# Mixture-of-experts kernel: gate logits carried through the attention, expert rows gathered by a table

## The chip, the cores and the metric

One core of one Trainium2 chip. The metric is the device time of one run in microseconds, the median of several runs. The kernel before has 408.28 us (three runs, 408.23 to 409.46).

## What is computed

Three stages follow each other. A linear attention with a decaying state gives 1536 tokens of 384 features (2 batches, 8 heads, 768 positions, 48 features a head). A mixture of experts sends each token to the expert with its largest logit, at most 384 tokens an expert, in order of the tokens. A dense layer with h - tanh(h) follows.

```python
for t in range(S):                               # attention
    cur = einsum('bhd,bhe->bhde', u[None] * kt, vt)
    y[:, :, t] = einsum('bhd,bhde->bhe', rt, state + cur)
    state = w[None, :, :, None] * state + einsum('bhd,bhe->bhde', kt, vt)
...
logits = x @ w_gate                              # experts: N=1536, D=384, E=8, F=1024
expert_idx = argmax(logits, axis=1)
gate_w = softmax(logits)[arange(N), expert_idx]
for i in range(N):
    e = expert_idx[i]
    if counts[e] < capacity:
        disp[e, counts[e]] = x[i]; pos[i] = counts[e]; counts[e] += 1; keep[i] = True
h = maximum(einsum('ecd,edf->ecf', disp, w1), 0)
y = einsum('ecf,efd->ecd', h, w2)
out[i] = gate_w[i] * y[expert_idx[i], pos[i]]    # where kept
...
h = x @ w_in; out = (h - tanh(h)) @ w_out        # dense, d_ff = 2048
```

## The kernel before

**Attention.** Twelve steps n, each a tile of 128 tokens of all eight heads; steps 0 to 5 are the first batch, 6 to 11 the second. TensorE runs in each step, in the order of its program: score products into pA (L1140, L1144), the state update pT (L1165, not in steps 5 and 11), queries times state (L1174) and later scores times values (L1189) into pY, the "own" products with u for the next step (`own_products`, L1105), the transposes of the x of the step before (`x_transposed`, L1084), the transposed own rows (`own_transposed`, L1116), and the logits of the step before (`logits`, L1094). VectorE writes the weighted queries (`queries`, L792), the masked scores (L880), the weighted keys (`keys`, L784), the state (L890, L892) and x (`output`, L859). GpSimd multiplies r and k (`products`, L481), makes the keys for the state (`end_keys`, L489) and v times the own term (vdiag, L507). ScalarE scales queries and state, and copies out of PSUM. SP issues the loads (`feature_part`, `token_part`, `value_part`).

**Routing.** Tiles are routed in groups, 4, 4, 2, 2. `route1` finds a tile's expert from the logits, `route2` the gate and the place in the expert; ROUTE1, ROUTE2, SCALED and SENT say in which step that, the scaling of x by the gate (`scale_x`, ScalarE) and the sending happen. Groups 2 and 3 come at the end of the attention. x goes to the tensor x_by_slot in HBM, where a row's address is its expert and place: ScalarE fills it with zeros by nine transfers of 576 KB (L650), GpSimd scatters the rows of each tile by an indirect DMA (`scatter`, L472). SP loads an expert's 384 rows by one plain transfer (`expert_rows`).

**Between attention and experts.** Rows of tiles 0 to 7 for expert 0 are loaded (`loaded`, L1211). Those of tiles 8 to 11 are taken straight from SBUF: VectorE writes one-hot matrices (`spots_of`, L837) and TensorE multiplies x by them (`direct`, L1205). ScalarE and VectorE split the result in a high and a low part (`split_x`, L939).

**Experts.** For each expert TensorE does `first` (three products of high and low parts for each block), transposes the next expert's rows (`transposed_rows`, L1254), and does `second`. Weights go HBM to four raw buffers, ScalarE makes the high part (L580), VectorE the low part of W1 (L849), GpSimd that of W2 (`low`, L460). In experts 0 and 1 GpSimd also scatters six tiles' token numbers each by rank (`token_ranks`, L521). Each engine runs its own instructions in the order of its program; all order between engines is by semaphores written by hand.

The steps of the prediction touch these names and lines, the queue of GpSimd above all.

Of the kernel before, what the change touches and what calls it, by code (L numbers as in the profile page):

```python
# [21 lines left out]
ALU = mybir.AluOpType  # L22
# [7 lines left out]
P = 128  # L30
# [10 lines left out]
REF = 32  # L41
KD = D // P
# [5 lines left out]
XS = 10  # L48
# [5 lines left out]
ZP = 9  # L54
# [11 lines left out]
def build(nc, by_feature_d, by_token_d, w_d, u_d, wg_d, w1_d, w2_d, out_d):  # L66
    xs_d = nc.dram_tensor("x_by_slot", (E * CAP + N, D), F32, kind="Internal").ap()
# [3 lines left out]
    with ctx:  # L71
# [26 lines left out]
        limit = sb("slot_limit", [P, GS], F32)  # L98
# [4 lines left out]
        sloti = sb("sloti", [P, NG, GS], I32)  # L103
# [14 lines left out]
        large_i = sb("large_i", [P, 1], I32)  # L118

# [3 lines left out]
        kv = sb("kv", [P, 3, 2, D], F32, att)  # L123
# [7 lines left out]
        vdiag = sb("vdiag", [P, D], F32, att)  # L131
        diag = sb("diag", [P, 2, H], F32, att)
        own_rows_sb = sb("own_by_head", [P, P], F32, att)
        st = sb("st", [P, 2, NP, DH], F32, att)
        stw = sb("stw", [P, NP, DH], F32, att)
        x = sb("x", [P, XS, D], F32, att)
        xT = sb("xT", [P, KD, P], F32, att)
        early = sb("early", [P, 1], F32, att)
        wcol = sb("wcol", [P, NP], F32, att)
        ucol = sb("ucol", [P, NP, 2], F32, att)  # L140
        wgate = sb("wgate", [P, KD, E], F32, att)
        pw = sb("powers", [P, NP, 2 * REF + P], F32, att)
        kendt = sb("kendt", [P, NP, 2, HALF], F32, att)
# [3 lines left out]
        zero_row = x[:, XS - 1, :]  # L147
# [38 lines left out]
        u_in = sem("u_in")  # L186
        wgate_in = sem("wgate_in")
        feature_in = [sem(f"feature_in{i}") for i in range(3)]
        token_in = [sem(f"token_in{i}") for i in range(3)]
# [8 lines left out]
        xs_zero = sem("xs_zero")  # L198
# [20 lines left out]
        lg_full = sem("lg_full")  # L219
        lg_done = sem("lg_done")  # L220
# [3 lines left out]
        xt_full = sem("xt_full")  # L224
        xt_done = sem("xt_done")
# [10 lines left out]
        scat = [sem(f"scattered{i}") for i in range(STEPS)]  # L236
# [93 lines left out]

        def place(n):
# [6 lines left out]
        def expert_rows(e):  # L338
            return xs_d[bass.ds(e * CAP, CAP), :].rearrange("(b p) d -> p b d", p=P)
# [12 lines left out]
        def _(sp):  # L352

            def feature_part(n):
                if n < 3:
                    sp.dma_start(rkT[:, n], by_feature_d[n]).then_inc(feature_in[n], 16)
                else:
                    sp.wait_ge(e_ready, n - 2)
                    sp.wait_ge(kw_ready, n - 2)
                    sp.wait_ge(rk_ready, n - 2)  # L360
                    for par in range(2):
                        rows = slice(par * HALF, par * HALF + DH)
                        sp.dma_start(rkT[rows, n % 3], by_feature_d[n, rows]).then_inc(feature_in[n % 3], 16)

            def token_part(n):
# [4 lines left out]
                sp.dma_start(kv[:, n % 3, 0], by_token_d[n, :, 0]).then_inc(token_in[n % 3], 16)  # L370

            def value_part(n):
# [4 lines left out]
                sp.dma_start(kv[:, s, 1], by_token_d[n, :, 1]).then_inc(value_in[s], 16)  # L377
# [11 lines left out]
            sp.dma_start(ucol[:, :, :], u_d).then_inc(u_in, 16)  # L389
# [4 lines left out]
            sp.dma_start(wgate[:, :, :], wg_d.rearrange("(c p) e -> p c e", p=P)).then_inc(wgate_in, 16)  # L394
# [12 lines left out]
            unit(2, 0, 0)  # L407
            unit(2, 0, 1)
# [980 lines left out]
```

## Time and profile before

| what | value |
|---|---|
| median of three runs | 408.28 us |
| the profiled execution, its own time | 410.51 us |
| its span, first to last instruction | 408.8 us |
| TensorE busy | 384.9 us, 94% |
| VectorE busy | 214.2 us, 52% |
| ScalarE busy | 180.9 us, 44% |
| GpSimd busy | 155.7 us, 38% |
| granted TensorE clock, mean | 0.980 |
| moved by DMA | 56.85 MB, 139 GB/s |

PE is TensorE's product, PEld its weight load, DVE VectorE, ACT ScalarE, POOL GpSimd, SP SyncE. The granted clock is a share of 2.4 GHz; 0.50 is 1.2 GHz. The shares are means over the whole span; the stages differ much.

### The profile page before, as it was taken

To read this page: it belongs to the slowest core of one execution; us is meant where nothing else is said; L and a number is where in the kernel's file an instruction comes from. 1 tells how busy PE (TensorE), PEld (TensorE's weight loads), DVE (VectorE), ACT (ScalarE), POOL (GpSimd) and SP (SyncE) were. 2 spreads that over 40 slices of the span, in tenths; PEclk is the share of its full clock that TensorE was granted. 3 is DMA by queue.
4 is the path that set the end of the run, shared out by engine and by line. 5 is a ranking of instruction groups with operands and counts; after the bars stand their busy time and mean duration, and the time that the engine had idled before them with its cause. 6 is when DMAs were issued, how large, how long until landed. Compare 5 with 4: busy or idle time off the path is not lost.

```text
span 408.8 us, 10468 instructions
## 1 busy us (share of the span) xinstructions
PE 384.9 (94%) x3738; PEld 373.1 (91%) x3739; DVE 214.2 (52%) x453; ACT 180.9 (44%) x486; POOL 155.7 (38%) x132
## 2 busy tenths in 40 slices
PE   7999898698999999999999899999999999999991
PEld 7777687598999999999999899999999999999991
DVE  7667978574555655555465356615252434343340
ACT  5553456434564665756656454533022313231220
POOL 3966665435877742715517051541002000110002
PEclk9999999689999999999999999999999999999997
DMA  7989986444849478576684527000000000010001
GB/s 246 271 251 269 249 211 220 141 149 154 264 162 285 150 249 261 189 253 192 224 284 158 182 79 226 6 21 38 0 0 19 38 0 0 0 58 0 0 0 65
DMA packets 41541, 56.85 MB, mean 139 GB/s; under 512 B 3584, under 2 KB 39104, under 8 KB 41504
## 3 DMA queue, kind: packets, MB, share of 16 engines
q1 hardware_dynamic: 35936, 46.23, 36.9%
q10 hardware_dynamic: 3600, 5.31, 4.1%
q0 software_dynamic: 1968, 4.83, 3.1%
q8 instruction: 22, 0.36, 0.4%
q14 instruction: 15, 0.12, 0.1%
HBM read 46.23 MB, written 10.13 MB: 138 GB/s over the span
## 4 chain that ended last, share of the span: by engine, by line
PE 58%; issue 18%; POOL 13%; DVE 4%; DMA 2%; ACT 2%; another core or an unknown queue 1%; POOLq 0%; DVEq 0%; SPq 0%; ACTq 0%
POOL w_lo L460 11%; PE ring L1065 9%; PE ring L1067 9%; PE ring L1066 9%; PE pO L1317 8%; PE pO L1316 8%; PE pY L1189 2%; POOL token_of_rank L521 2%; PE ring L1205 2%; PE pA L1140 2%; PE pD L1094 1%; DVE At L880 1%; PE pY L1174 1%; PE pX L1084 1%
## 5 line engine op out<-in xcount | busy, mean ns | idle before, releaser
L460 POOL TENSOR_TENSOR w_lo<-raw_weights,w_hi 128x768 fp32r<-128x768 f32 x40 | 73.5, 1846 | 84.6 <-ACT w_hi L580 84.3
L1007 DVE SCALAR_TENSOR_TENSOR minus_tanh<-square,ring 128x384 f32<-128x384 f32 x64 | 35.5, 554 | 93.5 <-ACT square L730 79.1
L580 ACT ACTIVATE w_hi<-raw_weights 128x768 fp32r<-128x768 f32 x80 | 67.1, 848 | 28.5 <-DMA raw_weights<-w 28.4
L730 ACT ACTIVATE square<-ring 128x384 f32<-128x384 f32 x64 | 31.4, 491 | 94.7 <-DVE h_hi L1017 53.8
L1065 PE MATMUL ring<-yT_hi,w_hi 128*128 x192 | 65.0, 339 | 1.7 <-DVEq L1002 1.7
L1316 PE MATMUL pO<-w_hi,h_hi 128*128 128x384 f32 x192 | 64.9, 338 | 0.0
L1317 PE MATMUL pO<-w_lo,h_hi 128*128 128x384 f32 x192 | 64.8, 338 | 0.0
L1066 PE MATMUL ring<-yT_lo,w_hi 128*128 x192 | 64.8, 338 | 0.0
L1067 PE MATMUL ring<-yT_hi,w_lo 128*128 x192 | 64.8, 338 | 0.0
L1065 PE MATMUL ring<-xT_hi,w_hi 128*128 128x224 f32 x192 | 52.9, 275 | 1.6 <-issue 1.1
L849 DVE TENSOR_TENSOR w_lo<-raw_weights,w_hi 128x768 fp32r<-128x768 f32 x40 | 42.4, 1073 | 22.3 <-ACT w_hi L580 18.7
L550 POOL DMA_INDIRECT out<-out_rows,tok x12 | 11.7, 976 | 111.1 <-ACT out_rows L725 107.2
L1065 PE MATMUL pO<-h_hi,w_hi 128*128 128x224 f32 x192 | 53.2, 277 | 0.0
L1067 PE MATMUL ring<-xT_hi,w_lo 128*128 128x224 f32 x192 | 52.6, 274 | 0.6 <-issue 0.6
L1066 PE MATMUL ring<-xT_lo,w_hi 128*128 128x224 f32 x192 | 52.6, 274 | 0.0
L1067 PE MATMUL pO<-h_hi,w_lo 128*128 128x224 f32 x192 | 52.6, 274 | 0.0
L1066 PE MATMUL pO<-h_lo,w_hi 128*128 128x224 f32 x192 | 52.6, 274 | 0.0
L967 DVE SCALAR_TENSOR_TENSOR h_lo<-ring,h_hi 128x224 fp32r<-128x224 f32 x64 | 24.3, 390 | 32.9 <-ACT h_hi L697 30.9
L1065 PEld LDWEIGHTS ring<-xT_hi,w_hi 128*128 128x128 f32 x192 | 36.8, 192 | 2.8 <-issue 2.0
L1065 PEld LDWEIGHTS ring<-yT_hi,w_hi 128*128 128x128 f32 x192 | 36.0, 188 | 1.9 <-issue 1.9
L1065 PEld LDWEIGHTS pO<-h_hi,w_hi 128*128 128x128 f32 x192 | 36.8, 192 | 0.1
L1067 PEld LDWEIGHTS pO<-h_hi,w_lo 128*128 128x128 f32 x192 | 36.9, 192 | 0.0
(158 smaller groups left out, 744.1 us busy)
## 6 DMA issues: line engine op xcount, KB each, us to landing
raw_weights<-w SPq DMA_DIRECT2D x80, 384.0 KB
x_by_slot<-x ACTq DMA_DIRECT2D x9, 576.0 KB, 4.4
x_expert<-x_by_slot SPq DMA_DIRECT2D x8, 576.0 KB
kv<-kv_by_token SPq DMA_DIRECT2D x22, 192.0 KB, 4.2
rkT<-rk_by_feature SPq DMA_DIRECT2D x18, 192.0 KB, 5.1
rkT<-rk_by_feature SPq DMA_DIRECT2D x3, 512.0 KB, 4.5
x_expert<-x_by_slot SPq DMA_DIRECT2D x1, 384.0 KB
x_by_slot<-x,sloti POOLq DMA_INDIRECT x12, 4.1
```

The lines of the kernel that those rows point to most:

```text
L460: pool.tensor_tensor(lo, unit_raw(2, k), hi.bitcast(F32), ALU.subtract).then_inc(w2_ready, 1)
L550: pool.indirect_dma_start(out=out_d, out_offset=bass.IndirectOffsetOnAxis(ap=tok3[:, i:i + 1], axis=0), in_=ost[:, i, :], in_offset=None). ...
L580: act.activation(hi, unit_raw(what, k), ACT.Copy).then_inc(w1_hi if what == 1 else w2_hi, 1)
L730: act.activation(sq[:, i % 2, :], ring[i % 4][:, 0:CAP], ACT.Square, scale=THIRD ** 0.5, accum_out=sqsum[:, bass.ds(t * (2 * FC) + i, 1)]) ...
L849: dve.tensor_tensor(lo, unit_raw(1, k), hi.bitcast(F32), ALU.subtract).then_inc(w1_ready, 1)
L967: dve.scalar_tensor_tensor(out=hl[:, f, 0:cols], in0=ring[f % 4][:, 0:cols], scalar=0.0, in1=hh[:, f, 0:cols].bitcast(F32), op0=ALU.max, o ...
L1007: dve.scalar_tensor_tensor(out=nt[:, i % 2, :], in0=sq[:, i % 2, :], scalar=1.0, in1=ring[i % 4][:, 0:CAP], op0=ALU.subtract, op1=ALU.mult ...
L1065: pe.matmul(out, hi, m_hi, start=first, stop=False)
L1066: pe.matmul(out, hi, m_lo, start=False, stop=False)
L1067: return pe.matmul(out, lo, m_hi, start=False, stop=last)
L1316: pe.matmul(pO[k][:, 0:D], g, W2h[:, s, f, :], start=starts, stop=False)
L1317: last = pe.matmul(pO[k][:, 0:D], g, W2l[:, s, f, :], start=False, stop=(ends and not general))
```

## The change

The logits are no longer computed from the finished x. The gate's weights multiply v ahead of the attention (together with the own products, with v by feature as one more input), and each head's eight logits stand behind its 48 values, in a row of 64 with room (`gated_values`). The attention carries them as it does the values, so that x comes out as 56 columns a head, and VectorE sums the eight logits over the heads (`owners_of`). The transposes of x, the logit products and their copies go.

x is stored by token (x_d, SP, twelve plain transfers) and not by slot; the zero fill goes but for one row. A table of the row of each slot is made by products of one-hot matrices (`tabled`), the matrices by GpSimd for tiles 0 to 3, one tile in each of steps 8 to 11 (`spread`, SPREAD), and by VectorE for the others. GpSimd gathers the rows of every expert by three indirect DMAs (`gather`, `expert_rows`). These stand in GpSimd's order behind the low parts and the rank scatters of an expert.

The routing groups are 4, 4, 4. The work of a group is cut in four pieces (`owners_of`, `counts_of`, `route2`, `places_of`) in different steps. The low parts of W1 of expert 0 move behind the attention.

```diff
-GROUPS = [(0, 4), (4, 4), (8, 2), (10, 2)]
+GROUPS = [(0, 4), (4, 4), (8, 4)]
-ROUTE1 = {5: 0, 9: 1}
+OWNERS = {4: 0, 8: 1}
+COUNTS = {5: 0, 9: 1}
 ROUTE2 = {6: 0, 10: 1}
-SCALED = {8: [0, 1], 9: [2, 3], 11: [4, 5, 6, 7]}
-SENT = {9: [0, 1], 10: [2, 3], 11: [4, 5, 6, 7]}
+PLACES = {7: 0}
+SPREAD = {8: 0, 9: 1, 10: 2, 11: 3}
+SCALED = {7: [0], 8: [1], 9: [2], 10: [3], 11: [4, 5, 6, 7]}
...
@@ sync
-            for n in range(DIRECT):
-                sp.wait_ge(scat[n], 16)
-            sp.dma_start(xe[:, 0:2, :], expert_rows(0)[:, 0:2, :]).then_inc(xe_in, 16)
...
+            for n in range(STEPS):
+                sp.wait_ge(xg_ready, n + 1)
+                sp.dma_start(x_d[1 + n * P:1 + (n + 1) * P, :], row(n)).then_inc(stored[n], 16)
+            for k in range(4):
+                unit(2, 0, k)
             with sp.Fori(0, E - 1) as e:
                 for k in range(4):
                     unit(1, e + 1, k)
-                sp.wait_ge(ring_full, e * RING + (RING + KD))
-                sp.dma_start(xe[:, :, :], expert_rows(e + 2)).then_inc(xe_in, 16)
...
@@ gpsimd
+            def spread(n):
+
+                pool.wait_ge(places_ready, 1)
+                pool.tensor_scalar(qhot[:, n, :], counts[:, :], reached[:, n:n + 1], tokno[:, n:n + 1], ALU.is_equal, ALU.mult)
+                pool.tensor_scalar(phot[:, n, :], lanes[:, :], lane_no[:, n:n + 1], None, ALU.is_equal
+                                   ).then_inc(pool_hot_ready, 1)
...
+            def gather(source, rows, k, landed):
+
+                pool.sem_inc(passed, 1)
+                pool.indirect_dma_start(
+                    out=xe[:, k, :], out_offset=None, in_=source,
+                    in_offset=bass.IndirectOffsetOnAxis(ap=rows[:, k:k + 1], axis=0)).then_inc(landed, 16)
+
+            def expert_rows(e):
+
+                pool.tensor_copy(row3[:, :], row_i[:, e, :]).then_inc(row3_made, 1)
+                pool.wait_ge(row3_made, e)
+                for k in range(BLOCKS):
+                    gather(x_d, row3, k, xe_in)
...
                 for n in range(e * C, (e + 1) * C):
                     token_ranks(n)
-            with pool.Fori(1, E // 2 + 1) as j:
+                pool.wait_ge(ring_full, e * RING + (RING + KD))
+                expert_rows(e + 2)
...
@@ vector
+                gated = x[:, first % XS:first % XS + m, :].rearrange("p i (h e) -> p i e h", h=H)
+                link(dve.tensor_reduce(logit[:, 0:m], gated[:, :, DH:DV, :], AX.X, ALU.add))
...
+                if n == STEPS - 1:
+                    places_of(1, rlink)
...
+            spread(1)
             output(STEPS - 1)
+            owners_of(2, rlink)
+            counts_of(2, rlink)
             route2(2, rlink)
-            spots_of(8)
...
+            for n in range(DIRECT, STEPS):
+                spots_of(n)
+            places_of(2, rlink)
+            spread(2)
+            low(0, 0, 0)
...
@@ tensor, own_products
+                    pe.matmul(pX[32 * p:32 * p + 2 * E + 2, D:D + P], own_gate[:, 0, p, :], rkf[:, p, :],
+                              start=True, stop=False, skip_group_check=True)
+                pe.wait_ge(vfeature_in[n % 3], loaded_features(n))
+                for p in range(NP):
+                    last = pe.matmul(pX[32 * p:32 * p + 2 * E + 2, D:D + P], own_gate[:, 1, p, :], vT[:, n % 3, p, :],
+                                     start=False, stop=True, skip_group_check=True)
...
+            pe.wait_ge(pool_hot_ready, DIRECT // 2)
+            pe.wait_ge(hot_ready, 1)
+            tabled(range(DIRECT))
+            pe.wait_ge(diag_ready, STEPS)
+            keep_warm(8, ones[:, :], pX[:, 0:P])
+            pe.wait_ge(x_ready, STEPS)
+            positions(2)
```

## Rows read from the trace of the kernel before

**Rows 1.** Windows by stage: length, busy us of each engine (instructions), clock, DMA share, GB/s
```profile
14.70:70.40 55.70, 51.22 (x1265) 43.07 (x1264) 44.80 (x87) 29.04 (x117) 36.81 (x32) 1.00 0.84 239
...
92.90:228.90 136.00, 134.92 (x1200) 134.20 (x1200) 74.30 (x147) 82.43 (x175) 73.08 (x45) 1.00 0.69 219
```

**Rows 2.** Chain of waits, one attention step: start us, length us, what
```profile
25.97 0.21 PE pA L1140
...
26.99 0.60 PE pT L1165 x16
27.59 0.61 PE pY L1174 x32
28.20 0.33 PE pX L1105 x8
28.54 0.48 PE pX L1084 x3
29.01 1.07 PE pY L1189 x32
...
30.34 0.57 PE pD L1094 x6
```

**Rows 3.** Timeline and groups of instructions, GpSimd in the attention
```profile
28.71 1.37 POOL L481 TENSOR_TENSOR rkf<-rkT 128x512 f32<-128x512 f32 x1 [1.47 <-PE pX L1105]
...
35.42 1.01 POOL L489 TENSOR_TENSOR kend<-kv,kendt 128x384 f32<-128x384 f32 x1
...
L489 POOL TENSOR_TENSOR kend<-kv,kendt 128x384 f32<-128x384 f32 x8 | 9.8, 1226 | 0.0
```

**Rows 4.** Timeline, VectorE, routing in the attention
```profile
39.49 1.07 DVE L800 TENSOR_TENSOR ldiff<-logit,lmax 128x32 f32<-128x32 f32 x1
...
61.27 0.18 DVE L799 TENSOR_REDUCE lmax<-logit 128x4 f32<-128x32 f32 x1
61.48 0.19 DVE L800 TENSOR_TENSOR ldiff<-logit,lmax 128x32 f32<-128x32 f32 x1
```

**Rows 5.** Timeline, TensorE, from the last attention step to the experts
```profile
72.92 1.14 PE L1189 MATMUL pY<-kv,At 128*64 128x48 f32 x32 [0.52 <-DVE At L880]
...
80.93 4.08 PE L1205 MATMUL ring<-kw,x 128*128 128x224 f32 x10
...
86.69 1.48 PE L1211 MATMUL ring<-ident,x_expert 128*128 128x128 f32 x12
88.00 2.46 PE L1205 MATMUL ring<-At,x 128*128 128x224 f32 x12
...
92.94 0.36 PE L1065 MATMUL ring<-xT_hi,w_hi 128*128 128x224 f32 x1 [1.14 <-issue]
```

**Rows 6.** Timeline, VectorE, the same stretch
```profile
77.48 0.55 DVE L859 TENSOR_TENSOR x<-vdiag,pY 128x384 f32<-128x384 f32 x1 [2.03 <-remote]
...
79.22 0.75 DVE L837 TENSOR_SCALAR kw<-At,token_slot 128x384 f32<-128x384 f32 x2
...
90.51 0.99 DVE L939 TENSOR_TENSOR xT_lo<-ring,xT_hi 128x224 fp32r<-128x224 f32 x3
```

**Rows 7.** Timeline, GpSimd, in experts 0 and 1
```profile
105.16 1.52 POOL L521 DMA_INDIRECT token_of_rank<-tokrow,rank_i  x1
...
112.39 0.96 POOL L521 DMA_INDIRECT token_of_rank<-tokrow,rank_i  x1 [0.30 <-issue]
115.67 7.26 POOL L460 TENSOR_TENSOR w_lo<-raw_weights,w_hi 128x768 fp32r<-128x768 f32 x4 [2.32 <-ACT w_hi L580]
...
130.86 0.96 POOL L521 DMA_INDIRECT token_of_rank<-tokrow,rank_i  x1 [0.30 <-issue]
```

**Rows 8.** Timeline of TensorE, and GpSimd's scatters of x by tile
```profile
136.43 0.82 PE L1254 MATMUL ring<-ident,x_expert 128*128 128x128 f32 x6
...
DMA to landing us min/median/max: 3.3/4.1/7.3
```

**Rows 9.** Windows of one microsecond, columns as in the first group
```profile
75.00:76.00 1.00, 0.80 (x6) 0.70 (x6) 0.45 (x1) 0.00 (x0) 0.93 (x1) 0.69 0.52 197
```

More of the change, by code:

```diff
@@ L41 @@
 REF = 32
+DV = DH + E
+WIDE = HALF
+BLOCKS = CAP // P
+Q = E * BLOCKS
 KD = D // P
@@ L513, in _ @@
                               allow_small_or_imprecise_dtypes=True).then_inc(slots_ready, 1)
-                for i in SENT.get(n, []):
-                    scatter(i)
-            for n in range(DIRECT, STEPS):
-                scatter(n)
+                if n in SPREAD:
+                    spread(SPREAD[n])
+            def gather(source, rows, k, landed):
[8 more added lines that the diff above has]
+                    gather(x_d, row3, k, xe_in)
+            pool.wait_ge(table_done, 1)
+            link(pool.tensor_copy(early_i[:, :], table[:, 0, 0:BLOCKS]))
+            pool.wait_ge(zero_in, 16)
+            for n in range(DIRECT):
+                pool.wait_ge(stored[n], 16)
+            gather(x_d[0:1 + DIRECT * P, :], early_i, 0, xe_in)
+            gather(x_d[0:1 + DIRECT * P, :], early_i, 1, xe_in)
+            gather(x_d[0:1 + DIRECT * P, :], early_i, 2, xe_rest_in)
+            pool.wait_ge(table_done, 2)
+            link(pool.tensor_tensor(table[:, 2, :], table[:, 0, :], table[:, 1, :], ALU.add))
+            link(pool.tensor_copy(row_i[:, 0:E, :].rearrange("p e k -> p (e k)"), table[:, 2, :]))
+            for n in range(DIRECT, STEPS):
+                pool.wait_ge(stored[n], 16)
+            pool.wait_ge(xe_rest_in, 16)
+            pool.wait_ge(ring_full, KD)
+            pool.wait_ge(meta_ready, 1)
+            with pool.If(tokens_of(pool, 0) > NARROW):
+                pool.wait_ge(wide_full, KD)
+            expert_rows(1)
             def token_ranks(n):
@@ L535, in _ @@
                         low(j * 2 + s, k, s)
+                    pool.wait_ge(ring_full, (j * 2 + s) * RING + (RING + KD))
+                    pool.tensor_copy(row3[:, :], row_i[:, bass.ds(j * 2 + (s + 2), 1), :].rearrange("p a k -> p (a k)")
+                                     ).then_inc(row3_made, 1)
+                    pool.wait_ge(row3_made, j * 2 + (s + 2))
+                    for k in range(BLOCKS):
+                        gather(x_d, row3, k, xe_in)
+            for e in range(E - 2, E + 2):
+                for k in range(4):
+                    low(e, k, e % 2)
+                if e == E - 2:
+                    pool.wait_ge(ring_full, e * RING + (RING + KD))
+                    expert_rows(E)
             pool.wait_ge(rank_sc, STEPS * 16)
@@ L622, in decayed_state, with table_copy @@
                     last.then_inc(stw_ready, 1)
+            def table_copy(g):
+                act.wait_ge(table_full, g + 1)
+                act.copy(table[:, g, :], pD[:, 0:Q]).then_inc(table_done, 1)
             def decayed_queries(n):
@@ L809, in route1, with counts_of @@
                                        bc(owners.unsqueeze(2), [P, m, E]), ALU.is_equal))
+            def counts_of(g, link):
+                first, m = GROUPS[g]
+                owners = allf[:, 0, first:first + m]
                 for i in range(m):
@@ L1125, in positions, with tabled @@
                           start=False, stop=True).then_inc(pos_full, 1)
+            def tabled(tiles):
+                for n in tiles:
+                    last = pe.matmul(pD[:, 0:Q], phot[:, n % DIRECT, :], qhot[:, n % DIRECT, :], start=(n == tiles[0]),
+                                     stop=(n == tiles[-1]))
+                last.then_inc(table_full, 1)
             for n in range(STEPS):
```

348 lines of the change are left out of this document (158 added, 190 removed).

## The prediction

> **What bounds the kernel now.** I read the windows view first, cut where the work changes. From 14.7 to 70.4 us run the attention steps 1 to 10 (step n begins with its score products): TensorE is busy 51.2 of 55.7 us, VectorE 44.8, GpSimd 36.8, and the DMA engines 84%. From 92.9 to 228.9 us the eight experts run with TensorE busy 134.9 of 136.0 us; behind them lies the dense part, which the change leaves alone. So whatever is won ahead of the experts shortens the run, unless an expert then has to wait [rows 1]. The chain of waits gives one undisturbed attention step: scores from 25.97, state update 0.60, state times queries 0.61, own products 0.33, transposes of x 0.48, values 1.07, own transpose, logits 0.57 ending at 30.91, so 4.94 us of TensorE without a hole [rows 2]. Ten steps of it are 49.4 us of the 55.7; the other 6.3 us are late VectorE work around the routing and short holes. Then comes the piece between attention and experts: the last value products start at 72.92 and end at 74.06, the first expert product starts at 92.94. I call these points Y (end of the last value products) and F. F minus Y is 18.9 us [rows 5].
>
> **Profiled run and median.** Its span is 408.8 us and its own time 410.51 us, the median of the runs 408.28 us. The sum below is made in that span as a difference, and goes onto the median.
>
> **The attention step.** Removed from TensorE: the transposes of x (0.48) and the logits (0.57). Added: the own products now also take four products with v, as many as there were, so 0.33 more [rows 2]. The operands of state and value products widen from 48 to 64 columns. The records do not scale with columns there: the 32 value products take 33 ns each start to start, two at a time on different columns of the array, and the full-width score products run beside the 64-column ones in the same time. I take 0 for the widening; the other bound is a third of 0.60 + 0.61 + 1.07, that is 0.76 us a step. TensorE is then at 4.94 - 0.48 - 0.57 + 0.33 = 4.22 us. But something else is late next. GpSimd starts the r times k product 0.18 us after the own products end (28.53 to 28.71), its end-keys follow 1.2 us later and take 1.01, or 1.23 on average, and the state update waits for them [rows 2, 3]. That loop is 0.18 + 1.2 + 1.01 + 0.1 + 0.60 + 0.61 + 0.66 = 4.36 us, 4.6 with the mean duration. I take 4.5 us a step, 45 for ten; bounds 4.36 and 4.98 (TensorE with the whole widening).
>
> GpSimd also gets the one-hot rows of a tile in each of steps 8 to 11, two single-input operations of 24 and 128 columns. Nothing in the trace has that form on GpSimd; the nearest are its 1.37 us for 512 columns with two inputs and 1.01 for 384 [rows 3], so 0.3 to 0.7 us together. They stand ahead of the next r times k product, but GpSimd has a hole there, and I count them at nothing; without the hole they would cost 4 times 0.7 at most.
>
> VectorE: x is 448 instead of 384 wide, under 0.1 us. Routing comes in pieces after the state copy. A small operation takes 0.18 us and the next starts 0.21 later, but one that meets GpSimd took 1.07 [rows 4]. Owners of four tiles is now seven operations with the added sum over heads, about 2.0 us; counts, gates and places about 1.2 each. The hole after the state copy in a 4.5 us step is about 1.1 us (VectorE busy 44.8 of 55.7 us now). So each owners piece puts 0.9 us on the path, about 1.7 with a collision like the 1.07, and the others 0.2 to 0.4: 4.5 us for all. Short holes of the kind seen now I keep at 3 us. The front grows 0.5 us through the longer own products and five more constants. Step 11 needs 0.9 us more, since the places of the second group stand ahead of its score copy. Sum: 45 + 4.5 + 3 + 0.5 + 0.9 = 53.9 against 55.7: **-1.8 us** to Y (from -5 to +3 with the bounds). The zero fill leaves 9 transfers of 576 KB off the DMA engines, 5.3 MB, against 3.2 MB of v twice more; both ride on queues that no step waits for now, so 0. SP issues two more transfers a step and the stores of x, all inside its idle time, since it waits for the steps.
>
> The Trainium skill, "SBUF — State Buffer", section "Who interferes with whom", says that a VectorE operation with two SBUF inputs and a GpSimd one that reads SBUF block each other. The 1.07 us fits. By that rule alone each of the spread routing pieces could wait for one GpSimd operation, which makes the attention about 5 us longer than my sum.
>
> **Between Y and F.** Now VectorE writes x only at 77.48 after 2.03 us of waiting for something unnamed [rows 6], and GpSimd was then sending rows out; those scatters go. The new order from Y: x done Y+0.75; owners, then counts Y+3.3; position products, Y+4.1; positions summed Y+4.6; four spot matrices at 0.375 each (0.75 for two) [rows 6]: Y+6.1. TensorE starts the gathering products at Y+5.2. It has 24 records of 224 columns (12 products), and 12 took 2.46 us at full clock [rows 5], so Y+9.9; then the products with the loaded rows, 1.48 for 12 [rows 5], Y+11.2. The two gathers of loaded rows start on GpSimd at about Y+3 and land by Y+8.5, in time. VectorE goes on from Y+6.1: places 1.2, one-hots 1.2, w low part 0.9, counts 1.7, tail values 0.6, w low part 0.9, three splits of 0.33 [rows 6], so Y+13.8. TensorE needs the table products, 4 warm products and 1.1 us for the branch: F = Y+14.4. Against 18.9 this is **-4.5 us**. Two low parts of W1 that now ride inside the attention are counted here, and the two behind F end before the fifth block of the first expert asks for them.
>
> **Behind F.** Expert rows now come by three GpSimd gathers each, not by one transfer from SP. They stand in GpSimd's queue behind the low parts of W2 and, in experts 0 and 1, behind six scatters of token ranks each; queued behind them are the next low parts, which TensorE's second products need. Now: six ranks from 105.16 to 113.35, low parts 115.67 to 122.93, six ranks up to 131.82 [rows 7]. New, counted from F (92.94 now): ranks end F+20.4; three gathers at 1.3 us apart to F+24.6, in a hole of which 2.3 us were free; low parts 7.3, F+31.9; six ranks 8.8, F+40.7; a copy and a wait 0.4; the last gather starts F+43.7. A scatter of the same 192 KB lands 3.3 to 7.3 us after its start, median 4.1 [rows 8], so the rows are there at F+47.8. TensorE wants them for the transposes of expert 3 at 136.43, F+43.5 [rows 8]. Nothing behind can give this back, as TensorE has 1.1 idle us in 136 [rows 1]. So **+4.3 us** (3.5 to 7.5), about 1 of it already at expert 2. From expert 4 on GpSimd has no ranks, and its 7.3 + 4.3 us fit into the 16.7 of an expert.
>
> The Trainium skill, "DMA: Bandwidth & Descriptors", section "Anatomy of one DMA — SWDGE (gpsimd) path", gives 2.0 us and the bytes over 436 GB/s, 2.45 us for such a gather. Its landing would then be F+46.2 and the stall 2.7 us, and the result 404.8 us. The 4.1 of the trace decides here.
>
> **Sum.** -1.8 - 4.5 + 4.3 = -2.0; 408.3 - 2.0 = **406.3 us**.
>
> **Rivals.**
> - *The clock falls again behind Y.* Now it falls within 75 to 76 us (mean 0.69 in that microsecond, so from 2.4 to 1.2 GHz inside it), after some 3.5 us in which TensorE had only 1.1 us of full products and small ones, and records of the gathering products then take 0.41 us [rows 5, 9]. The new stretch has 1.9 idle us ahead of the value products (late score copy), 1.1 us of them, then 24-column table products, and only then eight warm ones. For the fall: so little work. Against: the stretch is some 2 us shorter. Price: positions about 2 us later behind slow warm products, and gathering records at 0.41 us each (10 took 4.08) instead of 0.205 (12 took 2.46) [rows 5] for some of them, 1 to 3 us: +3.5 us, so 409.8 us. It decides once the clock is at 1.2 GHz before Y+3.
> - *Slower: VectorE and GpSimd become the bound of the attention.* If a collision meets most routing pieces and the widening costs its 0.76, Y is not 1.8 us earlier but 3 later: -2.0 + 4.8 gives 411.1 us. It decides when the step passes 5.1 us. For: the 1.07 for 0.19 us. Against: the widened records are not bound by columns.
> - *The gathers are covered.* If they land in 2.5 us and the ranks in their shortest spacing, the stall is 2 us, and with a step at 4.36 the result is 402.6 us. For: fewer bytes on the queues. Against: nothing in rows 8 is under 3.3.
>
> **Chances.** My forecast's case 0.37, the clock 0.25, the slow attention 0.18, the covered gathers 0.20. About 0.3% (1.2 us) is what a measurement of this kernel can tell from no change. The forecast's own case scatters by 2 us, so 0.24 of it lies below 407.1 and the rest near none; the covered gathers are faster in full; of the clock 0.06 is within and 0.19 slower; the slow attention is slower but for 0.03. Faster 0.44, same 0.22, slower 0.34. Range: 402.0 to 412.5, which leaves out the outer parts of the last two cases.
>
> **What would show it.** Steps 1 to 4 at 4.4 to 4.6 us with the state update waiting for GpSimd's end-keys; VectorE full in steps 4 and 8; clock at 1.0 through Y+3 to Y+11; F some 14 us behind Y; TensorE idle before the transposes of experts 2 (about 1 us) and 3 (about 3), released by an indirect transfer, and nowhere else among the experts. Wrong if the wide products lengthen the step, if the ranks leave room for the gathers, or if the clock falls.

## The result and the profile after

The changed kernel takes 416.73 us (median of four, 414.48 to 419.38), the kernel before 408.25 us beside it (four, 405.47 to 409.46). The ratio is 1.022, with a 95% interval of 1.013 to 1.031: slower by 8.5 us, where 2 us faster had been forecast, and outside the forecast range.

The profiled execution took 418.18 us, the one of the kernel before 410.51 us; each column of the table below is one execution. Three points carry the comparison, all read from TensorE's timeline: Y, the end of the last value products; F, the first expert product; and D, the first product of the dense part. D stands at 230.6 us before and at 238.51 after.

| us | before | after | difference | forecast |
|---|---|---|---|---|
| Y | 74.06 | 76.16 | +2.1 | -1.8 |
| F minus Y | 18.88 | 15.74 | -3.1 | -4.5 |
| D minus F | 137.7 | 146.6 | +8.9 | +4.3 |
| behind D | 178.2 | 177.9 | -0.3 | 0 |
| sum (spans 408.8 and 416.4) | | | +7.6 | -2.0 |

First the stages of the kernel after (windows: stretch, length, busy us of TensorE, its weight loads, VectorE, ScalarE, GpSimd with instructions, clock, DMA share, GB/s), to be laid beside [rows 1]:

```profile
14.70:70.40 55.70, 46.77 (x1246) 37.98 (x1244) 49.17 (x85) 25.64 (x107) 38.48 (x35) 0.97 0.73 196
...
92.90:228.90 136.00, 129.53 (x1126) 128.69 (x1124) 72.64 (x145) 79.57 (x166) 101.78 (x75) 0.97 0.68 209
```

In the attention TensorE works 4.5 us less in the same window and VectorE 4.4 us more; among the experts TensorE, busy 134.9 of 136.0 us before, is now idle or slow, and GpSimd's busy time rises from 73.1 to 101.8 us. The largest waits of TensorE that are new or have grown are these (total us, times, longest):

```profile
PE ring L1317 <- DMA x_expert<-x_by_token,row: 5.5, 2, 3.7
PE pY L1256 <- DVE At L953: 4.3, 6, 2.0
PE pY L1245 <- issue: 3.3, 3, 1.5
```

**Among the experts.** The rows arrive by a transfer, so the transfer is named. The chain of waits that ended last (each piece followed back to what released it) names the real cause. From just ahead of F it leaves TensorE and stays in GpSimd's queue for 46 us (start, length, what; the longest pieces):

```profile
92.24 0.90 POOL row L543
...
98.07 7.23 POOL w_lo L484 x4
105.47 1.54 POOL token_of_rank L570
...
119.22 7.11 POOL w_lo L484 x4
126.50 1.53 POOL token_of_rank L570
...
138.60 3.85 DMA x_expert<-x_by_token,row
142.57 1.43 PE ring L1317 x6
```

Low parts, six rank scatters, three gathers; again low parts, scatters, gathers; then one gather's landing, and TensorE. A full turn of this queue takes 21.0 us (105.47 to 126.50), while TensorE turns an expert round in 16.7 once nothing disturbs it (transposes of two later experts at 160.99 and 177.72). So the queue loses 4.3 us in each turn with rank scatters. What reaches TensorE is read from its transposes. Those of expert 2 come at F+30.4 instead of F+26.3 (119.20 us before), 4.1 us late, and those of expert 3 at F+50.7 instead of F+43.5, 7.2 us late (timeline; the wait is in brackets):

```profile
122.26 1.54 PE L1317 MATMUL ring<-ident,x_expert 128*128 128x128 f32 x6 [3.72 <-DMA x_expert<-x_by_token,row]
...
142.57 1.43 PE L1317 MATMUL ring<-ident,x_expert 128*128 128x128 f32 x6 [1.75 <-DMA x_expert<-x_by_token,row]
```

**The clock behind a wait.** The granted clock, a share of 2.4 GHz, falls when work comes back. Windows of one microsecond behind the second wait:

```profile
142.00:143.00 1.00, 0.43 (x3) 0.44 (x4) 0.00 (x0) 0.00 (x0) 1.00 (x1) 0.86 0.12 28
143.00:144.00 1.00, 1.00 (x7) 1.00 (x5) 0.40 (x2) 0.69 (x2) 1.00 (x2) 0.50 0.99 340
...
146.00:147.00 1.00, 1.00 (x10) 1.00 (x10) 1.00 (x1) 0.14 (x1) 1.00 (x2) 0.93 0.67 207
```

The engine sat idle from 140.8 to 142.6 us and then ran at 1.2 GHz for some 3.2 us. Summing what the windows fall short of 1.00 gives 1.7 us, and the next transposes come 18.4 us later (142.57 to 160.99) instead of 16.7: the same 1.7. With the 7.2 us above this gives the 8.9 of the table. The fall behind the first wait is as deep, but adds nothing, since GpSimd's queue sets the time of the second wait anyway.

**In the attention.** The start of VectorE's masked-score copy marks the steps. From step 4 to step 10 it takes 33.6 us before (32.01 to 65.63) and 34.9 after. The five profiles that have this attention (this one and those of experiments 1, 3, 4 and 5 below) lie between 34.8 and 35.5 us, the two that have the attention before at 33.2 and 33.6, so this difference is clear of the scatter. Y is not as firm: 77.35 us in the second profile of the attention before, where the clock was at 0.50 from 26 to 32 us. VectorE's timeline after:

```profile
32.17 1.31 DVE L953 COPY_PREDICATED At<-before,pA 128x1024 f32<-128x1024 uint32 x1
...
40.35 2.60 DVE L867 TENSOR_TENSOR upto<-upto,onehot 128x8 f32<-128x8 f32 x4
...
59.23 0.80 DVE L854 SCALAR_TENSOR_TENSOR score<-ldiff,prio 128x32 f32<-128x32 f32 x1 [0.16 <-DVE ldiff L851]
...
63.79 1.89 DVE L867 TENSOR_TENSOR upto<-upto,onehot 128x8 f32<-128x8 f32 x4
...
67.08 1.29 DVE L953 COPY_PREDICATED At<-before,pA 128x1024 f32<-128x1024 uint32 x1
```

Four additions of eight columns take 2.60 and 1.89 us here. The first such chain took 0.77 us in the kernel before (at 42.00), and it takes 0.77 behind the attention of this one (78.77), where GpSimd is nearly idle. The chain of waits has the four additions singly, and GpSimd's timeline what it ran beside them:

```profile
40.43 1.17 DVE upto L867
...
41.62 0.94 DVE upto L867
...
42.58 0.18 DVE upto L867
```

```profile
39.90 1.66 POOL L491 TENSOR_TENSOR rkf<-rkT 128x512 f32<-128x512 f32 x1 [0.48 <-PE pX L1166]
41.52 1.00 POOL L499 TENSOR_TENSOR kend<-k_tok,kendt 128x384 f32<-128x384 f32 x1
```

The first addition ends at 41.60, GpSimd's product at 41.56; the second ends at 42.56, GpSimd's end-keys at 42.52. With GpSimd idle behind them the others take 0.18 us. From 45 to 60 us VectorE has no room left:

```profile
45.00:60.00 15.00, 12.14 (x331) 9.90 (x331) 14.50 (x27) 8.04 (x35) 11.68 (x11) 1.00 0.71 171
```

It is busy 14.50 of 15 us, where it was 12.69 before, and TensorE is busy only 12.14. In the first steps the changed kernel loses what it had gained: TensorE has a hole of 1.53 us at 17.07 ("issue", no releaser in the trace), the clock is at 0.50 from 20 to 23 us, and at step 4 the two kernels are level (32.01 and 32.17). Where the hole is missing, in experiment 9, step 4 begins at 30.82. A hole of 1.47 us at 66.95 is followed by no fall of the clock.

**Between Y and F.** TensorE's timeline, to be laid beside [rows 5]:

```profile
75.01 1.15 PE L1256 MATMUL pY<-v_and_gate,At 128*64 128x64 f32 x32 [1.96 <-DVE At L953]
...
78.19 3.50 PE L1146 MATMUL pX<-ones 128*128 128x128 f32 x16
...
83.02 2.54 PE L1266 MATMUL ring<-kw,x 128*128 128x224 f32 x12 [0.75 <-DVE kw L915]
85.39 2.43 PE L1266 MATMUL ring<-At,x 128*128 128x224 f32 x12
87.66 1.47 PE L1272 MATMUL ring<-ident,x_expert 128*128 128x128 f32 x12
...
91.90 0.37 PE L1138 MATMUL ring<-xT_hi,w_hi 128*128 128x224 f32 x1 [0.51 <-DVE xT_lo L1010]
```

The gathering products run at full speed, 12 in 2.54 and 2.43 us, where ten took 4.08. The warm products ahead of them ran at 1.2 GHz, 3.50 us for sixteen records. That fall cost a microsecond or so, as the runs below show by difference.

The 3.1 us won here should not be put down to the change alone. In the profile of before the clock is at 0.50 from 76 to 85 us, in that of after only from 78 to 81; summed as above, the fall takes 5.1 us of full clock there and 1.7 here, a difference as large as the gain. The stretch is also uneven from run to run in the kernel before: 20.7 us in experiment 2, and 14.4 in experiment 10, where Y was late and the fall behind it was short. What the change gives between Y and F at an equal clock is not shown.

### The profile page after: what moved, and what is told of

Read it like the earlier page. It is cut to its first block, busy times and chain, and to the rows that moved or that the text cites. A ratio compares the mean times of both kernels' runs of the same rounds, so it can differ in the third digit from the quotient of the medians.

```text
span 416.4 us, 10595 instructions
## 1 busy us (share of the span) xinstructions
PE 383.1 (92%) x3774; PEld 371.1 (89%) x3775; DVE 225.0 (54%) x454; ACT 178.0 (43%) x474; POOL 186.5 (45%) x171
## 4 chain that ended last, share of the span: by engine, by line
PE 70%; POOL 10%; DVE 10%; issue 5%; DMA 1%; ACT 1%; POOLq 0%; DVEq 0%; ACTq 0%
PE ring L1138 11%; PE ring L1139 11%; PE ring L1140 11%; PE pO L1379 8%; PE pO L1380 8%; PE pO L1139 4%; PE pO L1138 4%; PE pO L1140 4%; POOL token_of_rank L570 4%; POOL w_lo L484 3%; DVE At L953 2%; PE pY L1256 2%; POOL x_expert L537 1%; DVE rw L841 1%; DVE kw L833 1%
## 5 line engine op out<-in xcount | busy, mean ns | idle before, releaser
L1080 DVE SCALAR_TENSOR_TENSOR minus_tanh<-square,ring 128x384 f32<-128x384 f32 x64 | 35.5, 554 | 92.5 <-ACT square L779 92.5
L922 DVE TENSOR_TENSOR w_lo<-raw_weights,w_hi 128x768 fp32r<-128x768 f32 x40 | 43.4, 1099 | 20.8 <-ACT w_hi L643 20.2
L1138 PE MATMUL pO<-h_hi,w_hi 128*128 128x224 f32 x192 | 54.3, 283 | 0.0
L1139 PE MATMUL pO<-h_lo,w_hi 128*128 128x224 f32 x192 | 53.5, 279 | 0.0
L1138 PEld LDWEIGHTS pO<-h_hi,w_hi 128*128 128x128 f32 x192 | 38.0, 198 | 0.2 <-issue 0.2
L1138 PEld LDWEIGHTS ring<-yT_hi,w_hi 128*128 128x128 f32 x192 | 36.1, 188 | 2.1 <-issue 1.9
L1139 PEld LDWEIGHTS pO<-h_lo,w_hi 128*128 128x128 f32 x192 | 37.9, 198 | 0.0
```

The costliest lines, as they stand in the source:

```text
L922: dve.tensor_tensor(lo, unit_raw(1, k), hi.bitcast(F32), ALU.subtract).then_inc(w1_ready, 1)
L1080: dve.scalar_tensor_tensor(out=nt[:, i % 2, :], in0=sq[:, i % 2, :], scalar=1.0, in1=ring[i % 4][:, 0:CAP], op0=ALU.subtract, op1=ALU.mult ...
L1138: pe.matmul(out, hi, m_hi, start=first, stop=False)
L1139: pe.matmul(out, hi, m_lo, start=False, stop=False)
```

## The experiments

The theory by then: the time among the experts is lost because the gathers stand behind the rank scatters on GpSimd, and the time in the attention because VectorE is full, partly with operations that GpSimd makes slow. Ratios are to the kernel before on the same chip and carry the 95% interval. The scatter of single runs of either kernel is 1.5 to 2%, so the positions in the traces weigh more here than the medians.

**1. The rank scatters out of experts 0 and 1, in the changed kernel.**

```diff
-                if e == 0:
-                    pool.wait_ge(rank_ready, 1)
-                for n in range(e * C, (e + 1) * C):
-                    token_ranks(n)
                 pool.wait_ge(ring_full, e * RING + (RING + KD))
                 expert_rows(e + 2)
...
                 if e == E - 2:
                     pool.wait_ge(ring_full, e * RING + (RING + KD))
                     expert_rows(E)
+                    pool.wait_ge(rank_ready, 1)
+                for n in {E - 2: range(0, 2), E - 1: range(2, 8), E: range(8, STEPS)}.get(e, []):
+                    token_ranks(n)
```

> The changed kernel; only the twelve scatters of token ranks leave experts 0 and 1 on GpSimd's queue and run behind the low parts of experts 6, 7 and 8 (two, six, four). Theory (the expert rows are late because their gathers stand behind the rank scatters): no wait for a gather before the transposes, no fall of TensorE's clock among the experts, first expert product to first dense product 138 to 139 us instead of 146.6, the whole some 8 us under the changed kernel, 408 to 409.5 us, so level with the kernel before. Rival (three gathers an expert on GpSimd are too slow in themselves, or the stage is long for contention): the stretch stays over 142 us and the whole over 413.

Measured: 414.57 us against 413.33, ratio 1.0047 (1.0001 to 1.0092). From F (92.55) to D (231.36) 138.8 us instead of 146.6, and TensorE's waits hold none for the gathers. The 7.8 us are the scatters' place in the queue. By the ratios of this run and of the changed kernel (1.0047 and 1.022) the whole gains 1.7%, some 7 us.

**2. The same move in the kernel before.**

> The kernel before with the same move of the rank scatters. Its GpSimd has holes around them and nothing of TensorE waits for it, so the theory expects at most 1 us (its first two expert periods are 17.41 and 17.23 us against 16.72 later): 407 to 408.5 us. If rank scatters slow TensorE in themselves, through the DMA engines or ports, the two periods fall to 16.7 and the whole by more than 1 us.

Measured: 418.75 us, ratio 1.0118 (1.0044 to 1.0192), F to D 140.8 us. TensorE's period from expert 2 to expert 3 is 17.17 us, 17.23 before, so the scatters do not slow TensorE in themselves, and the move gains next to nothing where nobody waits for GpSimd, as expected. The loss was not expected. Part of it lies ahead of F (98.04 instead of 92.94), where the edit changes nothing and the clock was at 0.50 for longer (26 to 32 and 81 to 93 us). The other 3.1 us lie at the entry of the dense part:

```profile
234.31 0.35 ACT L709 CAST yT_hi<-pO 128x224 f32 x1 [1.54 <-PE pO L1070]
235.77 0.35 ACT L709 CAST yT_hi<-pO 128x224 f32 x1 [1.11 <-remote]
237.22 0.35 ACT L709 CAST yT_hi<-pO 128x224 f32 x1 [1.10 <-remote]
```

ScalarE's three copies of the last expert's result stand 1.45 us apart, while GpSimd issues six rank scatters from 228.14 to 236 us. Before they ran in 1.03 us together (from 228.37). What holds them ("remote", not an engine of the trace) is not settled; that it is the scatters is argued from the same time and from experiment 3.

**3. All twelve scatters in the dense part.** As 1, but with

```diff
-                for n in {E - 2: range(0, 2), E - 1: range(2, 8), E: range(8, STEPS)}.get(e, []):
+                for n in {E: range(0, 8), E + 1: range(8, STEPS)}.get(e, []):
```

> The changed kernel; all twelve rank scatters in the dense part, eight behind the low parts of its first half, four behind those of its second. With the scatters in experts 6 to 8 the three copies of expert 7's result came 0.3 to 0.7 us apart instead of at once and the stretch to the first dense product was 138.9. If indirect transfers being issued slow those copies, the stretch is now 137.5 to 138.2 us; if not, 138.9 again.

Measured: 411.83 against 410.99, ratio 1.0059 (1.0010 to 1.0107), F to D 137.1 us (92.49 to 229.62). The three copies run in 1.03 us again. So the whole difference among the experts is explained, and taken back, by the place of the scatters.

**4. As 3, with sixteen more warm records of TensorE ahead of the last value products.**

```diff
+                if n == STEPS - 1:
+                    keep_warm(8, ones[:, :], pD[:, P:2 * P])
                 pe.wait_ge(a_done, n + 1)
```

> The same, and TensorE runs eight warm products while it waits for the late score copy of step 11. Now its clock falls to 1.2 GHz from 77.9 to 81.1 us and the position products are ready only at 82.1, 2 us after VectorE asks for them. If idle time ahead of the last value products lets the clock fall, it stays at 1.0 here, the gathering products start about 1.7 us earlier and the first expert product comes 14 to 14.5 us behind the end of the last value products instead of 15.7. The rival, that the small table products behind it are what lets it fall, leaves 15.7. Whole: 1 to 3 us under the kernel before on the same chip if the first holds, level with it otherwise.

Measured: 410.81 us, ratio 0.9998 (0.9947 to 1.0048), level with the kernel before and not 1 to 3 us under it. The clock stays at 1.0 behind Y:

```profile
80.00:81.00 1.00, 1.00 (x11) 1.00 (x11) 0.93 (x3) 0.00 (x0) 0.00 (x0) 1.00 0.00 0
```

F minus Y is 14.7 us (79.61 to 94.27); Y itself is late, in part because the clock was at 0.79 from 60 to 76 us already, ahead of the edit, and in part because the new records (76.48 to 78.5) still ran when the score copy was done at 77.3. The experiment doesn't show that the warm records hold the clock: it also held behind Y in 3 and 5, without them. F minus Y is 14.6 and 14.3 there; in the changed kernel and in 1, where it fell, 15.7 and 15.9. The forecast 14.4 was right for the full clock, and the fall costs 1.3 us, not the 3.5 of the rival.

**5. The gathers ahead of the scatters.** Is it the order in the queue, or its length?

```diff
-                for n in range(e * C, (e + 1) * C):
-                    token_ranks(n)
                 pool.wait_ge(ring_full, e * RING + (RING + KD))
                 expert_rows(e + 2)
+                for n in range(e * C, (e + 1) * C):
+                    token_ranks(n)
```

> The changed kernel; in experts 0 and 1 the three gathers stand ahead of the six rank scatters instead of behind them. If the order alone is the trouble, the waits for gathers go and first expert product to first dense product falls to about 139 us, as with the scatters moved away. My theory says that the amount on GpSimd's queue is: four low parts 7.3, six scatters 9.2 and three gathers 4.2 us are 20.7 us in an expert of 16.7, so now the low parts of W2 of experts 1 and 2 come late, TensorE waits for them some 2 to 5 us in all, and the stretch is 141 to 144 us, against 146.6 with the gathers last.

Measured: 417.49 us, ratio 1.0178 (1.0080 to 1.0277), F to D 145.4 us. The gathers are in time, and no wait names them. But now the low parts behind the scatters are late, and TensorE waits for them:

```profile
140.82 0.37 PE L1138 MATMUL pO<-h_hi,w_hi 128*128 128x224 f32 x1 [2.96 <-POOL w_lo L484]
```

The clock is at 0.50 behind this wait too, from 142 to 144. Only 1.2 of the 8.9 us come back, less than the forecast of 141 to 144 us said. It is the length of the queue, not its order: 21.0 us of work against 16.7.

**6. GpSimd's one-hot rows behind the attention.** A rival of "VectorE is full" was that this new work of GpSimd slows the attention.

```diff
-                if n in SPREAD:
-                    spread(SPREAD[n])
...
+            for i in range(DIRECT // 2):
+                spread(i)
             pool.wait_ge(table_done, 1)
```

> The changed kernel; GpSimd makes the one-hot rows of tiles 0 to 3 behind the attention, not one tile in each of steps 8 to 11. It takes 1.5 us a step (0.46 and 1.0) ahead of the r times k product. If that delays the attention, the last value products end 2 us or more earlier than 76.2; if VectorE sets the pace there, as I think, they end under 1 us earlier, and the four tiles in a row (some 4.5 us) come out behind as a later table and no gain of the whole.

Measured: 420.57 us, ratio 1.0253 (1.0144 to 1.0362). Steps 4 to 10 take 34.8 us (34.9), and Y is at 76.6. F minus Y grows to 19.7 us, since the table products wait for the rows (2.0 us) and the clock is then at 0.50 from 78 to 84. One of the slow chains turns fast, as GpSimd is quiet there:

```profile
60.09 0.19 DVE L854 SCALAR_TENSOR_TENSOR score<-ldiff,prio 128x32 f32<-128x32 f32 x1 [0.16 <-DVE ldiff L851]
...
65.11 0.75 DVE L867 TENSOR_TENSOR upto<-upto,onehot 128x8 f32<-128x8 f32 x4
```

Yet the steps are no shorter: VectorE is busy 14.59 us from 45 to 60 as before. The collisions move to the key products (1.75 us at 63.11 for an operation that else takes 0.67), since the r times k product and the end-keys of GpSimd stay. The one-hot rows themselves are not the cause.

**7 and 8. One more operation of VectorE a step, in both kernels** (an unused reduction, in steps 1 to 10).

```diff
+                if 1 <= n <= 10:
+                    dve.tensor_reduce(spare[:, n, :], pw[:, :, 0:P], AX.X, ALU.max)
```

> The changed kernel with one more single-input VectorE operation (a maximum over 512 columns, about 0.6 us) behind the state copy in each of steps 1 to 10; its result is used by nothing. Theory (VectorE is the bound of the attention since the change): the end of the last value products moves from 76.2 us by 4 to 6 us, as only the first steps have a hole. Rival (the loop over GpSimd's end-keys or TensorE is the bound, VectorE has a hole of 1.1 us a step): it moves by under 2 us.

> The same additional VectorE operation in the kernel before. Theory (TensorE is the bound there, VectorE has a hole except in the routing steps): the end of the last value products moves from 74.1 us by under 2.5 us. If it moves by 4 to 6 as well, VectorE was the bound before already and the change's loss in the attention has to be read as VectorE work added to a full engine.

Measured: 421.75 us, ratio 1.0201 (1.0082 to 1.0321), and 418.63 us, ratio 1.0126 (0.9990 to 1.0262). Steps 4 to 10 grow by 1.2 us in both, from 34.9 to 36.1 and from 33.6 to 34.9, for six operations of 0.68, 4.1 us. Y moves by 3.0 and 1.9 us. By Y this did not tell the theories apart: it was to cost 4 to 6 us in the one and under 2.5 in the other. VectorE's busy time in steps 4 to 10 says more. In the changed kernel it grows by only 1.1 us (33.45 to 34.56), as other operations met GpSimd less (the two chains take 2.02 and 1.50 us, not 2.60 and 1.89), and the steps grow by as much. In the kernel before it grows by 2.8 us (28.23 to 31.01) and the steps by less than half of that. What VectorE is not busy in these six steps is 1.3 to 1.5 us in all nine profiles of changed kernels in this document, whatever was added or taken away, and 3.9 to 5.4 us in the four of the kernel before and its variants. In the changed kernel the steps follow VectorE.

**9 to 11. Less work for VectorE, with the same result.** The four chained additions of a group's running counts become a copy and a reduction over overlapping windows of five rows.

```diff
-        onehot = sb("onehot", [P, GS, E], F32)
+        window = sb("window", [P, 4 + GS, E], F32)
+        onehot = window[:, 4:4 + GS, :]
...
+            dve.memset(window[:, 0:3, :], 0.0)
...
-                for i in range(m):
-                    link(dve.tensor_tensor(upto[:, first + i + 1, :], upto[:, first + i, :], onehot[:, i, :], ALU.add))
+                link(dve.tensor_copy(window[:, 3, :], upto[:, first, :]))
+                five = window[:, 0:m, :]
+                five = bass.AP(five.tensor, five.offset, [five.ap[0], [E, m], [1, E], [E, 5]])
+                link(dve.tensor_reduce(upto[:, first + 1:first + m + 1, :], five, AX.X, ALU.add))
```

> The changed kernel, with the four chained additions of each group's running counts (in the trace of the changed kernel 2.60 us at 40.35 us and 1.89 us at 63.79 us, 0.77 us behind the attention) replaced by one copy and one reduction over overlapping windows, both with a single tensor input; an estimate for the two together is 0.6 us (a copy of 8 columns 0.17, a reduction of 96 to 128 columns 0.26 to 0.4). Nothing is left out. Theory VectorE sets the attention's pace in the changed kernel: about 3.3 us of its work go, and the last value products end 2.5 to 3.5 us earlier (73 to 74 instead of 76.2 us), the whole 2 to 3.5 us shorter. Rival, VectorE is only busy beside what sets the pace (TensorE with its clock, or the chain through ScalarE): the last value products end within 0.8 us of 76.2. First expert product to first dense product stays at 146 to 147 us by both.

> The kernel before with the same replacement (there the chains took 0.77 us at 42.00 and 1.76 us at 62.50 us, and 0.37 us each behind). Theory VectorE sets the pace only in the changed kernel: VectorE idles 1 to 3 us in every 15 us of this attention, and the end of the last value products moves by less than 0.8 us from 74.1; the whole within 1 us of the kernel before. Rival, VectorE sets the pace in both: 1.3 to 2 us earlier.

> The changed kernel with all twelve rank scatters in the dense part and the window reduction for the running counts. If both causes are the ones named and they add up: first expert product to first dense product 137 to 138 us, last value products at 73 to 75 us, and the whole 2 to 3 us below the version with only the scatters moved (which stood at 1.0059 of the kernel before), so about 0.995 to 1.000 of the kernel before. If VectorE is not what sets the attention's pace: 1.004 to 1.007 again.

Measured in the changed kernel: 414.95 us, ratio 1.0112 (1.0030 to 1.0193). Its VectorE:

```profile
30.82 1.32 DVE L957 COPY_PREDICATED At<-before,pA 128x1024 f32<-128x1024 uint32 x1
...
38.97 1.25 DVE L868 COPY window<-upto 128x8 f32<-128x8 f32 x1
40.26 0.45 DVE L871 TENSOR_REDUCE upto<-window 128x32 f32<-128x160 f32 x1
...
61.68 0.25 DVE L868 COPY window<-upto 128x8 f32<-128x8 f32 x1
61.96 0.44 DVE L871 TENSOR_REDUCE upto<-window 128x32 f32<-128x160 f32 x1
...
64.22 1.29 DVE L957 COPY_PREDICATED At<-before,pA 128x1024 f32<-128x1024 uint32 x1
```

The work went from 2.60 + 1.89 to 1.70 + 0.69 us, 2.1 less and not the 3.3 expected, because a copy with one input can meet GpSimd too (1.25 us). Steps 4 to 10 take 33.4 us, 1.5 less, which is what the kernel before needs (33.6). Y is at 74.09; 1.3 us of that gain are only the missing fall of the clock in the first steps (step 4 at 30.82). In the kernel before, the same edit leaves steps 4 to 10 at 33.9 us (33.21 to 67.10). So with less work for VectorE the steps get shorter in the changed kernel and not in the kernel before: VectorE is the bound after the change and was not before. The run of the kernel before is a weaker control than was meant, since one operation that met GpSimd (1.83 us at 62.77 for 0.19) took the saving away, and VectorE was busy 29.06 us in steps 4 to 10, not less than 28.23. From F to D this run took 143.4 us, less than the 146 to 147 expected. Its first low parts start at F+4.9 instead of F+6.2, several indirect transfers are issued in 1.0 instead of 1.6 us, and the clock holds behind the second wait (the waits are 2.38 and 1.39 us).

The kernel before with windows: 408.3 us, ratio 0.9928 (0.9882 to 0.9974), the fastest of all. Its Y was to stay within 0.8 us of 74.1 and is at 78.55, with the clock at 0.50 from 68.5 to 78; F is at 92.93, as before (92.94). The 3 us by which its profiled span is shorter lie behind D (175.7 us against 178.2), where the edit changes nothing: the products of the dense part take 334 ns each there and 338 in the profile before. So the gain of 0.7% is not shown to come from the windows. The changed kernel with windows and with all scatters in the dense part: 409.28 us, ratio 0.9959 (0.9924 to 0.9994), F to D 137.4 us, as expected, and steps 4 to 10 in 32.7. Y was expected at 73 to 75 us and is at 77.1, because TensorE stands still for 3.8 us ("issue") from 63.4 on in a step that VectorE, ScalarE and GpSimd wait through as well. F minus Y is 17.6 us there: TensorE waited 2.06 us for a gather of the first expert's rows, issued at 82.21 and there at 89.2, and the clock fell behind that wait (0.50 from 91 to 97). Both repairs together put the changed kernel 0.4% ahead of the kernel before. It remains behind or level with the kernel before once that has windows too.

## Why the prediction was wrong, step by step

**The gathers (+4.3 forecast, +8.9 measured).** The mechanism was right, the size was not. The prediction had the last of the second three gathers start at F+43.7; it starts at F+46.7 (138.60 - 91.90). Two of the three us are the gathers of expert 1, which it never put into the queue: they are issued from 93.93 to 98.06, and move the first low parts from F+4.2 (97.14 us in the kernel before) to F+6.2. This is the step that failed: the sum starts from "ranks end F+20.4", the time in the kernel before, where expert 1's rows need no gathers. The third is mostly the copy of the addresses and the wait ahead of each three gathers, 1.0 us each (114.65 to 115.67 and 135.01 to 136.03) instead of 0.3 and 0.4. The landing was right, 4.0 us against 4.1 [rows 8]. That makes the rows 7.2 us late instead of 4.3 (F+50.7 against F+43.5). The other 1.7 us were not in the sum: the clock after a wait, which the prediction had weighed behind Y only. 7.2 + 1.7 = 8.9. The estimate of 2.45 us for a gather from the Trainium skill, "DMA: Bandwidth & Descriptors", section "Anatomy of one DMA — SWDGE (gpsimd) path", does not fit among the experts: the gathers land 3.0 us after their issue at the least, 4.8 in the median. It does fit where the queues are nearly empty: the scatters of the result in the dense part, of the same 192 KB, land after 2.6 us in the median. (The case of that estimate would also give 404.7 us, not 404.8.)

**The attention (-1.8 forecast, +2.1 measured).** The terms of TensorE were right: the state products stay at about 0.6, the value products at 1.08 to 1.10 with 64 instead of 48 columns (1.07 before [rows 2]). But the step was not bound by TensorE or by the loop through GpSimd. The step that failed is the VectorE term. Its hole of "about 1.1 us in a 4.5 us step" was about right, as the five operations of every step take 3.3 us from start to start. The pieces that were to go into the hole were priced too low: "about 2.0 us" for owners and "about 1.2 each" for counts, gates and places. In steps 4 to 9 they take 3.1, 2.9, 1.2, 1.5, 2.9 and 2.2 us, 13.8 together instead of 8.8, and the running counts alone 2.60 and 1.89 us. Two key products that meet GpSimd (1.47 and 1.72 us for 0.67) come on top. With VectorE full, six steps take 5.8 us each. This is the rival "VectorE and GpSimd become the bound", near its price (Y 3 us later; measured 2.1) and without one of its conditions: the widening cost nothing. Its threshold of 5.1 us a step could not have told it from the forecast, since the kernel before has 5.6 us a step here. By the rule of the Trainium skill, "SBUF — State Buffer", section "Who interferes with whom", the prediction had estimated an attention 5 us longer than its sum; it came out 3.9 longer. The trace agrees with the rule in kind: the same operation at 0.19 or 0.80 us, the same chain at 0.77 or 2.60. The one-hot rows on GpSimd were forecast at 0.3 to 0.7 us and take 1.5 (0.44 and 1.06); that they cost the steps nothing was right, by experiment 6.

**Between Y and F (-4.5 forecast, -3.1 measured).** The length after the change was right to 0.3 us with the clock up (14.3 to 14.7 us in three runs, 14.4 forecast) and the first gathers in time; in the last run of experiment 11 they were not, and it is 17.6. The forecast's VectorE pieces add up to Y+13.6, not 13.8, which changes nothing. The base was weak: it took 18.9 us from one trace, with a wait of 2.03 us without a name and 10 us at the low clock in it. The rival of the clock came true at a third of its price, it seems because the fall caught the warm products and was over before the gathering products began.

**The sum.** None of the rivals held two of the three misses at once. The prediction gave each one its own case with the others at their forecast, and the range ended at 412.5; the three misses, 3.9, 4.6 and 1.3 us, all had the same sign. It also took 1.2 us, 0.3%, for what a measurement can tell; the ratio here is known to 0.9%.

**What stays open.** The holes that the trace puts down to "issue" or "remote": 1.5 us at 17.07 and 66.95 here, 3.8 us at 63.4 in the last run of experiment 11, 2.03 us in the kernel before [rows 6]. They stand in every run, at different places, and with the falls of the clock behind them they make up much of the scatter between runs. No experiment was aimed at them. Nor is it known whether windows help the kernel before.

## What to carry to other kernels

When work moves to an engine's queue, add up one whole turn of that queue, all it does in a period, and compare it with the period of the engine that it feeds; a turn that is longer is lost time as often as it repeats, in whatever order the queue stands. Work with a late deadline, here the rank scatters that only the dense part's end needs, belongs where the queue is empty. An engine busy for 85% whose operations grow beside another engine's does not have 15% to give: price its new operations at the duration that they have when they meet the other engine, and expect the bound to move to it. And where a forecast is a difference from one trace, look first at how much of the old stretch is a fallen clock or a hole without a name.

## What the runs showed of the hardware

- An idle TensorE can pay twice: behind waits of 3.72 and 1.75 us it ran at 1.2 GHz for some 3 us, worth 1.7 us each. Behind a wait of 1.39 us in another run, and behind a hole of 1.47 us in the attention of this one, the clock held.
- Two small VectorE additions that met GpSimd ended when its instructions did, at 41.60 and 42.56 us against 41.56 and 42.52. Small operations with GpSimd idle and beside it: 0.19 or 0.80 us, a chain of four 0.75 or up to 2.60 us, and a copy of eight columns with one input 0.17 or 1.25 us.
- GpSimd issues an indirect transfer of 128 rows in 0.95 us with 0.3 us between them, sometimes in 1.5 to 1.7.
- Indirect transfers of 192 KB from GpSimd land after 4.8 us in the median among the experts (gathers, DMA engines 68% busy) and after 2.6 us in the dense part (scatters, DMA engines 5% busy).
- While GpSimd issued six of them, ScalarE's copies of an expert's result stood 1.45 us apart instead of running in 1.03 us for all three; the cause is not shown.
